# The first attention iteration reordered: embedding chain behind it, table waits ahead of it, x transposes behind the state read

## The chip, the cores and the metric

The kernel runs on one core of a Trainium2 chip. The time is device time in microseconds (us) from start to end of one execution. A core has TensorE (PE in the profile; its weight loads are PEld), VectorE (DVE), ScalarE (ACT), GpSimd (POOL) and SyncE (SP). Each works through its own list of instructions in order and meets the others at semaphores: a wait stops everything behind it on that engine. Transfers are issued by SP, ACT or POOL and run on 16 DMA engines.

## The reference

Three layers, all in float32. The data are x (8 batches, 8 heads, 512 tokens, 64) and a state of 32 rows per head.

```python
scores = scale * x @ state.T;   a = softmax(scores);   xread = a @ state
scores2 = scale * state @ x.T;  a2 = softmax(scores2); sread = a2 @ x
x = concat([xread, sread]).transpose(...).reshape(B * (S + Ns), H * D)      # 4352 rows of 512
en = expert_emb / |expert_emb|;  logits = (x / |x|) @ en.T / tau            # 8 experts
e = argmax(logits);  x = gate * (relu(x @ w1[e]) @ w2[e])
h = relu(x @ w_in);  out = (s * h * h + b) @ w_out
```

## The kernel before

The program has one stream per engine, written out by hand, and three stages: attention with routing, experts, dense layer.

**Attention.** A loop over the eight batches, `i` from 0 to 7. In iteration `i`, TensorE multiplies states by the transposed tokens (`scores`, L1263); ScalarE copies the result to `s_t`; VectorE takes its minimum `nb` (L971), ScalarE the exponential, TensorE turns it (`turn_e2`), ScalarE copies it to `a2_n` (L639), and `state_read` (L1319) multiplies it by x into `bank_r`. The other softmax goes over the turned scores in `bank_n`: VectorE subtracts the minimum, ScalarE takes the exponential (L659), VectorE sums and normalises (L994 to L1000). `x_transpose` (L1244) turns the tokens of the next batch in four pieces, two into each of two banks, and ScalarE's `x_evac` (L584) copies each to `x_t`. `token_read` of batch `i - 1` fills `x_rows`, which SP stores to `x_tok` in memory. Each iteration ends with a slice of the expert weights being split in two parts (`split_hi`, `split_lo`).

**Before the loop.** The states are turned in four groups by `st_transpose` and copied by VectorE's `evac_st` to `st_t`: group 0 ahead of the loop, the others in iteration 0. Group 3 and group 0 use `bank_r`, which `state_read` uses too. The expert embedding is normalised by a chain of 17 small steps (`embed`, the first on ScalarE at L644, the others on VectorE), turned by TensorE, and multiplied by the states (`embed_states`, L1280).

**Routing.** The logits of some batches together (groups 0,1,2 then 3,4 then 5, 6 and 7) are turned into positions: `choose` on VectorE, `ranks` on TensorE, `place` on VectorE, after which GpSimd scatters five columns of indices for each batch into `slot_tab` (L508). `ranks` of the group whose last batch is `b` runs in iteration `b + 2` and waits for the state logits of the batch before. The table is cleared first by a transfer from `zero_f` (L387), whose semaphore is `tab_cleared`. SP reads the first indices back (`idx_soon`, L400) once 25 scatters have landed, and its later stores stand behind that wait; then GpSimd gathers the rows of the first tile (L525).

**Order of transfers on SP:** x of batch 0 in eight pieces, states, x of batch 1, `w1[0]` (2 MB), x of batch 2, `w2[0]` (2 MB), two scalars, the clearing of the table, and then the loop's loads and stores.

**Waits on constants.** GpSimd makes the constants and raises `const_ready` and `tab_zero`. VectorE waits for `tab_zero` 8 (the last of GpSimd's writes) at the start of iteration 1.

Of the kernel before, what the change touches and what calls it, by code (L numbers as in the profile page):

```python
# [4 lines left out]
P = 128  # L5
# [6 lines left out]
def attention_moe_ffn(nc, x, state, emb, tau, w1, w2, w_in, w_out, s, b, out):  # L12
# [57 lines left out]
    with top:  # L70
# [400 lines left out]
        def _(pool):  # L471
# [23 lines left out]

            pool.wait_ge(tab_zero, 4)
            nc.gpsimd.memset(first_e[:], 0.0).then_inc(tab_zero, 1)
            pool.wait_ge(tab_zero, 5)
# [29 lines left out]

            pool.wait_ge(tab_cleared, 16)
            for bb in range(SOON):  # L530
# [47 lines left out]
        def _(act):  # L578
# [62 lines left out]

            x_evac(0, 0)
            act.wait_ge(emb_ready, 16)
            nc.scalar.activation(emb_sq[:], emb_sb[:], ACT.Square, accum_out=en[0:E, 0:1]).then_inc(emb_step, 1)  # L644
            for j in range(1, PAIRS):
                x_evac(0, j)
            for i in range(B):
                scores_evac(i)
                if i >= 1:
                    a1_evac(i - 1)  # L650
                exp_states(i)
                if i >= 1:
                    row_t_evac(i - 1)
                a2_evac(i)
                if i + 1 < B:
                    for j in range(2):
                        x_evac(i + 1, j)
                act.wait_ge(sh_done, i + 1)
                nc.scalar.activation(e1[:], e1[:], ACT.Exp, scale=-1.0).then_inc(e1_done, 1)  # L659
                if i + 1 < B:  # L660
                    for j in range(2, PAIRS):
                        x_evac(i + 1, j)
                if i >= 1:
                    rows_evac(i - 1)
                split_hi(i)
# [156 lines left out]
        def _(dve):  # L822
# [37 lines left out]

            def embed_turned():
                dve.wait_ge(emb_tr, 1)
                nc.vector.tensor_copy(emb_t[:], bank_l[:, L_SE:L_SE + PAIRS * E].rearrange("p (c e) -> p c e", e=E))\
                    .then_inc(emb_done, 1)

            def embed_states():
                dve.wait_ge(se_mm, 1)
                nc.vector.tensor_scalar(st_pair[:, :, :, P:P + E],
                                        bank_l[:, L_SE:L_SE + B * 2 * E].rearrange("p (b j e) -> p b j e", b=B, e=E),
                                        -1.0 / SCALE, None, ALU.mult).then_inc(se_ready, 1)  # L870
# [86 lines left out]
            e1_r = e1[:].rearrange("p t (h w) -> p (t h) w", w=NS)  # L957
            sc_r = bank_n[:].rearrange("p t (h w) -> p (t h) w", w=NS)
            dve.wait_ge(hot_zero, 5)
            embed()  # L960
            evac_st(0)
            embed_turned()
            for i in range(B):
                if i == 1:
                    dve.wait_ge(const_ready, CONSTS + 2)
                    dve.wait_ge(tab_zero, 8)
                for jj in range(2):
# [4 lines left out]
                if i >= 1:  # L972
                    a1_evac(i - 1)
                else:
                    for k in range(1, B // 2):
                        evac_st(k)
                dve.wait_ge(scN_done, i + 1)
# [24 lines left out]
                token_rows(i)  # L1002
                if i == 0:
                    embed_states()
                if i == B - 1:
# [225 lines left out]
        def _(pe):  # L1231
# [33 lines left out]

            def embed_turn():
                pe.wait_ge(emb_step, EMB_STEPS)
                for j in range(PAIRS):
                    last = nc.tensor.transpose(bank_l[:, L_SE + j * E:L_SE + (j + 1) * E], emb_n[:, j * P:(j + 1) * P], ident[0:E, 0:E])
                last.then_inc(emb_tr, 1)  # L1270

            def embed_states():
                pe.wait_ge(st_ready, B // 2)
                pe.wait_ge(emb_done, 1)
# [33 lines left out]
            def state_read(bb):  # L1308
                pe.wait_ge(a2_ready, 2 * bb + 2)
                if bb >= 1:  # L1310
                    pe.wait_ge(st_rows_ready, (P // NS) * bb)
                else:
                    pe.wait_ge(st_ready, B // 2)
                for jj in range(2):
# [74 lines left out]
            st_transpose(0)  # L1389
            embed_turn()  # L1390
            for i in range(B):
                scores(i)
                if i == 0:
                    for k in range(1, B // 2):
                        st_transpose(k)
                else:
                    turn_a1(i - 1)
                    turn_rows(i - 1)
                turn_scores(i)
                turn_e2(i)  # L1400
                if i == 0:
                    embed_states()
                else:
                    row_logits(i - 1)
                if i + 1 < B:
                    for j in range(2):
                        x_transpose(i + 1, j)
                state_read(i)
                if i + 1 < B:
                    for j in range(2, PAIRS):  # L1410
                        x_transpose(i + 1, j)
                for k in range(len(GROUPS)):
                    if GROUPS[k][-1] + 2 == i:
                        ranks(k, i)
                if i >= 1:
                    token_read(i - 1)
# [196 lines left out]
```

## Time and profile before

| | |
|---|---|
| median of 3 runs | 1444.6 us (1443.0 to 1444.9) |
| profiled execution | 1443.0 us, span from first to last instruction 1441.3 us |
| mean granted TensorE clock | 0.973 of full |
| busy | PE 1356.8 us, DVE 645.9, ACT 513.7, POOL 161.1 |
| attention and routing | to about 160 us of the span |

The share of an engine is an average over the three stages. What a change in the first stage is worth is read from that stage: the order in time of the instructions, what each waited for, and which event released the next stage.

### The profile page before, as it was taken

What the parts mean: (1) busy time and instruction counts of PE and PEld (TensorE: products, weight loads), DVE (VectorE), ACT (ScalarE), POOL (GpSimd) and SP (SyncE); (2) the same over time, 40 slices, a digit from 0 to 9 for tenths busy, and PEclk for the clock granted to TensorE, in tenths of its full rate; (3) what the DMA queues carried; (4) which work ended last, traced back from release to release, by engine and by line L of the source; (5) the groups of instructions that cost most, each with busy time, mean ns of one, the idle gap of its engine ahead of it and who ended that gap; (6) DMA issues with size and microseconds to landing.
All of it is one profiled execution on the core that took longest, in us unless ns stands there. A gap on an engine that the chain in (4) does not pass through costs nothing.

```text
span 1441.3 us, 22771 instructions
## 1 busy us (share of the span) xinstructions
PE 1356.8 (94%) x6908; PEld 1119.1 (78%) x6909; DVE 645.9 (45%) x1603; ACT 513.7 (36%) x953; POOL 161.1 (11%) x200
## 2 busy tenths in 40 slices
PE   7977579999999999997999999999999999999995
PEld 5756458888888878886888888888888888888884
DVE  5875353666664565557422423223232232322322
ACT  4864133555543454443422222222222222222221
POOL 1042410111110111115000101001010010100101
PEclk9997699999999999998999999999999999999998
DMA  9593451344441243141010100101000010000000
GB/s 252 157 110 53 84 189 38 114 165 176 142 152 45 99 166 118 45 176 44 8 37 1 59 0 19 39 0 58 0 29 29 0 58 0 32 26 0 30 0 30
DMA packets 75601, 100.20 MB, mean 70 GB/s; under 512 B 44424, under 2 KB 44968, under 8 KB 74544
## 3 DMA queue, kind: packets, MB, share of 16 engines
q1 hardware_dynamic: 62736, 69.71, 17.1%
q0 software_dynamic: 7200, 20.08, 4.2%
q10 hardware_dynamic: 5632, 9.98, 1.8%
q8 instruction: 20, 0.33, 0.1%
q14 instruction: 13, 0.11, 0.0%
HBM read 71.24 MB, written 28.66 MB: 69 GB/s over the span
## 4 chain that ended last, share of the span: by engine, by line
PE 79%; DVE 6%; DMA 4%; issue 4%; POOL 2%; ACT 1%; DVEq 1%; SPq 0%; ACTq 0%; POOLq 0%
PE bank_a L1544 26%; PE bank_n L1563 14%; PE bank_tt L1563 12%; PE bank_n L1497 11%; PE bank_a L1464 10%; DMA xg<-x_tok,g_idx 3%; POOL slot_tab L508 2%; PE bank_tt L1477 2%; DVE w_lo L1029 1%; PE bank_n L1446 1%; DMA slot_tab<-ids,pos_all 1%; DVE gc L834 1%; PE bank_a L1244 1%; DVE gc L836 1%; PE bank_r L1319 1%
## 5 line engine op out<-in xcount | busy, mean ns | idle before, releaser
L1191 DVE TENSOR_TENSOR sq<-rel 128x512 f32<-128x512 f32 (+1 forms) x144 | 95.5, 663 | 487.3 <-ACT rel L797 487.3
L797 ACT ACTIVATE rel<-bank_a 128x512 f32<-128x512 f32 (+1 forms) x144 | 82.8, 575 | 541.6 <-PE bank_a L1544 541.6
L1544 PE MATMUL bank_a<-y_hi,w_in_hi 128*128 128x512 f32 (+1 forms) x576 | 217.7, 378 | 0.1
L1544 PE MATMUL bank_a<-y_hi,w_in_lo 128*128 128x512 f32 (+1 forms) x576 | 217.3, 377 | 0.0
L1544 PE MATMUL bank_a<-y_lo,w_in_hi 128*128 128x512 f32 (+1 forms) x576 | 217.3, 377 | 0.0
L1497 PE MATMUL bank_n<-w_hi,hid_hi 128*128 128x512 f32 x296 | 118.0, 398 | 14.4 <-DVE hid_lo L1045 14.3
L1544 PEld LDWEIGHTS bank_a<-y_hi,w_in_hi 128*128 128x128 f32 x576 | 108.3, 188 | 21.4 <-issue 0.8
L1544 PEld LDWEIGHTS bank_a<-y_lo,w_in_hi 128*128 128x128 f32 x576 | 108.3, 188 | 20.7 <-issue 0.2
L1544 PEld LDWEIGHTS bank_a<-y_hi,w_in_lo 128*128 128x128 f32 x576 | 108.3, 188 | 19.9
L1497 PE MATMUL bank_n<-w_hi,hid_lo 128*128 128x512 f32 x296 | 116.9, 395 | 0.0
L568 POOL DMA_INDIRECT out_rows<-w_raw,out_id x34 | 36.5, 1074 | 691.8 <-DVE w_raw L1203 686.6
L1563 PE MATMUL bank_n<-wo_hi,g_hi 128*128 128x512 f32 x288 | 112.5, 391 | 0.7 <-DVE g_lo L1194 0.7
L1563 PE MATMUL bank_n<-wo_lo,g_hi 128*128 128x512 f32 x288 | 112.2, 390 | 0.0
L1563 PE MATMUL bank_n<-wo_hi,g_lo 128*128 128x512 f32 x288 | 112.1, 389 | 0.0
L1464 PE MATMUL bank_a<-w_hi,xg_hi 128*128 128x512 f32 x304 | 101.8, 417 | 3.4 <-DVE xg_lo L1016 2.8
L1563 PE MATMUL bank_tt<-wo_hi,g_hi 128*128 128x512 f32 x256 | 100.8, 394 | 0.0
L1563 PE MATMUL bank_tt<-wo_lo,g_hi 128*128 128x512 f32 x256 | 99.7, 389 | 0.0
L1563 PE MATMUL bank_tt<-wo_hi,g_lo 128*128 128x512 f32 x256 | 99.6, 389 | 0.0
L1194 DVE TENSOR_TENSOR g_lo<-sq,g_hi 128x512 fp32r<-128x512 f32 (+1 forms) x144 | 95.5, 663 | 6.8
L1464 PE MATMUL bank_a<-w_hi,xg_lo 128*128 128x512 f32 x304 | 97.5, 402 | 0.0
L801 ACT ACTIVATE g_hi<-rel 128x512 fp32r<-128x512 f32 (+1 forms) x144 | 87.7, 609 | 4.6
L1497 PEld LDWEIGHTS bank_n<-w_hi,hid_hi 128*128 128x128 f32 x296 | 56.7, 191 | 29.5 <-issue 15.0
(234 smaller groups left out, 2096.0 us busy)
## 6 DMA issues: line engine op xcount, KB each, us to landing
w_raw<-in_moe_w SPq DMA_DIRECT2D x16, 2048.0 KB, 9.3
moe_tok<-yg ACTq DMA_DIRECT2D x38, 256.0 KB, 2.0
x_tok<-x_rows SPq DMA_DIRECT2D x8, 1088.0 KB, 7.8
y_rows<-moe_tok SPq DMA_DIRECT2D x8, 1024.0 KB, 5.2
x_m<-in_x SPq DMA_DIRECT2D x7, 1024.0 KB, 8.4
win_raw<-in_moe_w_in SPq DMA_DIRECT2D x8, 512.0 KB, 10.6
w_raw<-in_moe_w_out SPq DMA_DIRECT2D x1, 4096.0 KB, 15.9
x_m<-in_x SPq DMA_DIRECT2D x8, 128.0 KB, 3.0
```

The costliest lines, as they stand in the source:

```text
L508: nc.gpsimd.indirect_dma_start(out=slot_tab[:, :], out_offset=bass.IndirectOffsetOnAxis(ap=pos_all[0:n, bb, t:t + 1], axis=0), in_=ids[0:n ...
L568: nc.gpsimd.indirect_dma_start(out=out[:, :], out_offset=bass.IndirectOffsetOnAxis(ap=out_id[:, r:r + 1], axis=0), in_=o_sb[:, k, :], in_o ...
L797: nc.scalar.activation(rel[:, k, 0:cols], ps_g[k][:, 0:cols], ACT.Relu).then_inc(rel_ready, 1)
L801: nc.scalar.activation(g_hi[:, k, 0:cols], rel[:, k, 0:cols], ACT.Square).then_inc(g_hi_done, 1)
L834: link(nc.vector.scalar_tensor_tensor(t, y, n2, y, ALU.mult, ALU.mult))
L1191: nc.vector.tensor_tensor(sq[:, 0:cols], rel[:, k, 0:cols], rel[:, k, 0:cols], ALU.mult).then_inc(sq_ready, 1)
L1194: nc.vector.tensor_tensor(g_lo[:, k, 0:cols], sq[:, 0:cols], g_hi[:, k, 0:cols], ALU.subtract).then_inc(g_ready, 1)
L1464: last = nc.tensor.matmul(ps_h[j][:], a[:, xc], w[:, c * F + j * BANK:c * F + (j + 1) * BANK], start=(c == 0 and a is xg_hi and w is w1_hi ...
L1477: last = nc.tensor.transpose(ps_ht[m][:, c * P:(c + 1) * P], hid[:, k * P:(k + 1) * P], ident[:])
L1497: last = nc.tensor.matmul(dst, a[:, kc], w[:, k * D:(k + 1) * D], start=(k == 0 and a is hid_hi and w is w2_hi), stop=(k == FC - 1 and w i ...
L1544: last = nc.tensor.matmul(ps_g[n % 2][:, 0:cols], w[:, wc], a[:, c, 0:cols], start=(c == 0 and w is w_in_hi and a is y_hi), stop=(c == DC ...
L1563: last = nc.tensor.matmul(ps_o[TROWS - rows + r], a[:, n % 2, rc], w[:, wc], start=(n == 0 and a is g_hi and w is wh), stop=(n == FC2 - 1 ...
```

## The change

On GpSimd the wait for `tab_cleared` moves ahead of the last four writes of constants. On VectorE the waits for `const_ready` and `tab_zero` 8 move from iteration 1 to ahead of iteration 0; `embed` and `embed_states`, now with the copy of the turned embedding in it, move to the end of iteration 0, and so does the evacuation of state group 3. On ScalarE the square of the embedding follows the first score evacuations. On TensorE the four x transposes all follow `state_read`, `ranks` precedes it, state group 3 is turned after the x transposes of iteration 0 and once the state rows have left `bank_r`, and the embedding's turn and products come after that, ahead of the scores of iteration 1. `state_read(0)` waits for one group of states instead of four.

```diff
--- before.py
+++ after.py
@@ -494,6 +494,7 @@
                            allow_small_or_imprecise_dtypes=True).then_inc(tab_zero, 1)
 
             pool.wait_ge(tab_zero, 4)
+            pool.wait_ge(tab_cleared, 16)
             nc.gpsimd.memset(first_e[:], 0.0).then_inc(tab_zero, 1)
             pool.wait_ge(tab_zero, 5)
             nc.gpsimd.memset(first_e[:, 0:1], 1.0).then_inc(tab_zero, 1)
@@ -526,7 +527,6 @@
                                              in_=x_tok[0:SOON * ROWS if isinstance(g, int) and g < EARLY else NTOK, :],
                                              in_offset=bass.IndirectOffsetOnAxis(ap=g_idx[:], axis=0)).then_inc(gathered, 16)
 
-            pool.wait_ge(tab_cleared, 16)
             for bb in range(SOON):
                 write_slots(bb)
             pool.wait_ge(soon_loaded, 16)
@@ -639,15 +639,15 @@
                     nc.scalar.activation(a2_n[:, :, jj * P:(jj + 1) * P], bank_t[jj].rearrange("p (t w) -> p t w", w=P),
                                          ACT.Copy).then_inc(a2_ready, 1)
 
-            x_evac(0, 0)
-            act.wait_ge(emb_ready, 16)
-            nc.scalar.activation(emb_sq[:], emb_sb[:], ACT.Square, accum_out=en[0:E, 0:1]).then_inc(emb_step, 1)
-            for j in range(1, PAIRS):
+            for j in range(PAIRS):
                 x_evac(0, j)
             for i in range(B):
                 scores_evac(i)
                 if i >= 1:
                     a1_evac(i - 1)
+                else:
+                    act.wait_ge(emb_ready, 16)
+                    nc.scalar.activation(emb_sq[:], emb_sb[:], ACT.Square, accum_out=en[0:E, 0:1]).then_inc(emb_step, 1)
                 exp_states(i)
                 if i >= 1:
                     row_t_evac(i - 1)
@@ -858,12 +858,10 @@
                 emb_link(nc.vector.tensor_scalar(emb_n[:], emb_sb[:], en[0:E, 5:6], inv_tau[0:E, :], ALU.mult, ALU.mult))
                 assert n_emb[0] == EMB_STEPS
 
-            def embed_turned():
+            def embed_states():
                 dve.wait_ge(emb_tr, 1)
                 nc.vector.tensor_copy(emb_t[:], bank_l[:, L_SE:L_SE + PAIRS * E].rearrange("p (c e) -> p c e", e=E))\
                     .then_inc(emb_done, 1)
-
-            def embed_states():
                 dve.wait_ge(se_mm, 1)
                 nc.vector.tensor_scalar(st_pair[:, :, :, P:P + E],
                                         bank_l[:, L_SE:L_SE + B * 2 * E].rearrange("p (b j e) -> p b j e", b=B, e=E),
@@ -956,14 +954,11 @@
 
             e1_r = e1[:].rearrange("p t (h w) -> p (t h) w", w=NS)
             sc_r = bank_n[:].rearrange("p t (h w) -> p (t h) w", w=NS)
+            evac_st(0)
+            dve.wait_ge(const_ready, CONSTS + 2)
             dve.wait_ge(hot_zero, 5)
-            embed()
-            evac_st(0)
-            embed_turned()
+            dve.wait_ge(tab_zero, 8)
             for i in range(B):
-                if i == 1:
-                    dve.wait_ge(const_ready, CONSTS + 2)
-                    dve.wait_ge(tab_zero, 8)
                 for jj in range(2):
                     dve.wait_ge(sT_ready, 2 * i + jj + 1)
                     if i >= 1:
@@ -972,8 +967,8 @@
                 if i >= 1:
                     a1_evac(i - 1)
                 else:
-                    for k in range(1, B // 2):
-                        evac_st(k)
+                    evac_st(1)
+                    evac_st(2)
                 dve.wait_ge(scN_done, i + 1)
                 nc.vector.tensor_reduce(m1[:], sc_r, X_AXIS, ALU.min).then_inc(m1_done, 1)
                 dve.wait_ge(m1_done, i + 1)
@@ -1001,6 +996,8 @@
                     .then_inc(a1_norm, 1)
                 token_rows(i)
                 if i == 0:
+                    evac_st(B // 2 - 1)
+                    embed()
                     embed_states()
                 if i == B - 1:
                     a1_evac(B - 1)
@@ -1263,14 +1260,11 @@
                         last = nc.tensor.matmul(bank_t[jj][p, :], st_t[:, i, jj, p], x_t[:, 2 * jj + par, :], start=True, stop=True)
                     last.then_inc(scT_done, 1)
 
-            def embed_turn():
+            def embed_states():
                 pe.wait_ge(emb_step, EMB_STEPS)
                 for j in range(PAIRS):
                     last = nc.tensor.transpose(bank_l[:, L_SE + j * E:L_SE + (j + 1) * E], emb_n[:, j * P:(j + 1) * P], ident[0:E, 0:E])
                 last.then_inc(emb_tr, 1)
-
-            def embed_states():
-                pe.wait_ge(st_ready, B // 2)
                 pe.wait_ge(emb_done, 1)
                 for bb in range(B):
                     for jj in range(2):
@@ -1310,7 +1304,7 @@
                 if bb >= 1:
                     pe.wait_ge(st_rows_ready, (P // NS) * bb)
                 else:
-                    pe.wait_ge(st_ready, B // 2)
+                    pe.wait_ge(st_ready, 1)
                 for jj in range(2):
                     for t in range(TPB):
                         for par in range(2):
@@ -1387,32 +1381,32 @@
                 x_transpose(0, j)
             pe.wait_ge(diag_ready, 16 * (P // NS))
             st_transpose(0)
-            embed_turn()
             for i in range(B):
                 scores(i)
                 if i == 0:
-                    for k in range(1, B // 2):
-                        st_transpose(k)
-                else:
+                    st_transpose(1)
+                    st_transpose(2)
+                if i >= 1:
                     turn_a1(i - 1)
                     turn_rows(i - 1)
                 turn_scores(i)
                 turn_e2(i)
-                if i == 0:
-                    embed_states()
-                else:
+                if i >= 1:
                     row_logits(i - 1)
-                if i + 1 < B:
-                    for j in range(2):
-                        x_transpose(i + 1, j)
-                state_read(i)
-                if i + 1 < B:
-                    for j in range(2, PAIRS):
-                        x_transpose(i + 1, j)
                 for k in range(len(GROUPS)):
                     if GROUPS[k][-1] + 2 == i:
                         ranks(k, i)
-                if i >= 1:
+                state_read(i)
+                if i + 1 < B:
+                    for j in range(PAIRS):
+                        x_transpose(i + 1, j)
+                if i == 0:
+                    pe.wait_ge(st_rows_ready, P // NS)
+                    st_transpose(3)
+                    pe.wait_ge(const_ready, CONSTS + 2)
+                    pe.wait_ge(st_ready, B // 2)
+                    embed_states()
+                else:
                     token_read(i - 1)
             turn_a1(B - 1)
             turn_rows(B - 1)
```

## Rows read from the trace of the kernel before

**Rows 1.** The page's busy time, share of the span and instructions of each engine.
```profile
PE 1356.8 (94%) x6908; PEld 1119.1 (78%) x6909; DVE 645.9 (45%) x1603; ACT 513.7 (36%) x953; POOL 161.1 (11%) x200
```

**Rows 2.** Timeline of the start: start us, us, engine, line, operation, idle before.
```profile
5.99 0.10 POOL L497 MEMSET first_e<- 128x8 f32 x1
...
6.38 0.10 POOL L502 MEMSET late<- 128x2 f32 x1
...
7.25 0.16 DVE L853 RECIPROCAL inv_tau<-inv_tau 128x1 f32<-128x1 f32 x1 [4.65 <-ACT emb_sq L644]
...
10.14 0.53 DVE L858 TENSOR_SCALAR emb_n<-emb_sb,en,inv_tau 8x512 f32<-8x512 f32 x1
...
13.54 0.18 DVE L863 COPY emb_t<-bank_l 128x32 f32<-128x32 f32 x1
...
13.77 3.68 PE L1263 MATMUL bank_tt<-x_t,st_t 128*64 128x512 f32 x8 [0.43 <-DVE st_t L841]
14.04 8.47 SPq L383 DMA_DIRECT2D w_raw<-in_moe_w  x1
...
16.41 0.69 DVE L971 TENSOR_REDUCE nb<-s_t 128x1 f32<-128x512 f32 x1 [2.69 <-ACT s_t L617]
...
21.61 2.04 PE L1280 MATMUL bank_l<-emb_t,st_t 128*64 128x8 f32 x64
...
23.94 0.91 SPq L387 DMA_DIRECT2D slot_tab<-zero_f  x1
...
32.06 1.27 DVE L971 TENSOR_REDUCE nb<-s_t 128x1 f32<-128x512 f32 x2
```

**Rows 3.** Transfers under way at 22 to 25 us, the last column us to landing.
```profile
w_raw<-in_moe_w SPq DMA_DIRECT2D x1, 2048.0 KB, 17.8
slot_tab<-zero_f SPq DMA_DIRECT2D x1, 144.0 KB, 9.7
```

**Rows 4.** Timeline of iteration 2, and rank matmuls of iteration 4.
```profile
44.73 1.27 DVE L971 TENSOR_REDUCE nb<-s_t 128x1 f32<-128x512 f32 x2
...
47.05 1.26 ACT L639 ACTIVATE a_n<-bank_tt 128x512 f32<-128x512 f32 x2
...
48.64 1.09 ACT L584 ACTIVATE x_t<-bank_a 128x512 f32<-128x512 f32 x2 [0.33 <-PE bank_a L1244]
...
48.97 1.97 PE L1319 MATMUL bank_r<-x_m,a_n 128*64 128x128 f32 x32
...
49.47 0.15 DVE L896 COPY st_rows<-bank_l 32x8 f32<-32x8 f32 x1
49.61 1.06 ACT L659 ACTIVATE e<-e 128x1024 f32<-128x1024 f32 x1
50.70 1.22 DVE L994 TENSOR_REDUCE s<-e 128x32 f32<-128x1024 f32 x1 [1.08 <-ACT e L659]
...
57.48 1.27 DVE L971 TENSOR_REDUCE nb<-s_t 128x1 f32<-128x512 f32 x2
...
78.89 0.59 PE L1380 MATMUL bank_l<-hot_g,ones_b 128*128 128x112 bf16 x14
```

**Rows 5.** Timeline of iteration 6 and its end.
```profile
100.97 1.27 DVE L971 TENSOR_REDUCE nb<-s_t 128x1 f32<-128x512 f32 x2
...
109.38 1.97 PE L1244 MATMUL bank_a<-ident,x_m 128*128 128x128 f32 x8 [5.11 <-DMA x_m<-in_x]
...
111.28 3.68 PE L1319 MATMUL bank_r<-x_m,a_n 128*64 128x128 f32 x32
...
117.61 0.98 POOL L508 DMA_INDIRECT slot_tab<-ids,pos_all  x1 [15.81 <-DVE pos_all L937]
...
119.78 0.33 SPq L392 DMA_DIRECT2D x_tok<-x_rows  x1
```

**Rows 6.** The chain that ended last, at the last scatter of group 1.
```profile
129.61 11.59 DMA slot_tab<-ids,pos_all
```

**Rows 7.** Transfers issued from 118 to 124 us, the last column us to landing.
```profile
x_tok<-x_rows SPq DMA_DIRECT2D x1, 1088.0 KB, 10.8
```

## The prediction

> **What bounds the kernel now.** I read the page's totals first [rows 1]: TensorE is busy for 94% of the span, so time is won or lost where TensorE waits, and a delay ahead of the expert and dense stages moves them whole. Then the timeline of the start [rows 2], the transfers that are on their way by then [rows 3], one plain iteration of the attention loop [rows 4], a later one that stalls [rows 5], and the hand-over from the loop to the experts: the chain [rows 6] and the store beside it [rows 7]. In the start the reader is to see that VectorE's first score reduction runs at 16.41 us and the embedding chain, 7.25 to 10.67, lies ahead of the state evacuation while TensorE waits for input. In rows 4, the reduction `nb` of one iteration at 44.73 and of the next at 57.48: a period of 12.75. In rows 6, the last slot-table scatter of group 1 lands 11.59 us after its issue and holds the chain; behind it come the early index load, the first gather and everything after it.
>
> **The change, part by part.** All times are shifts against the profiled execution (1443.0 us, span 1441.3).
>
> (a) The wait for the cleared table. GpSimd waits for the clearing transfer before its last four writes, and VectorE waits for the last of these (`tab_zero` 8) ahead of iteration 0. SyncE issues that transfer at 23.94, and no wait on computed data lies ahead of it in SyncE's queue, so the change does not move the issue [rows 2]. It takes 9.7 us to land [rows 3]: 33.6. The four writes take 6.48 - 5.99 = 0.5 [rows 2], hand-over 0.1: VectorE starts at 34.2 instead of 16.41, +17.8. Queued behind VectorE's wait are ScalarE's exponentials (they want `nb`), TensorE's transposes of `e2`, and so the state read. Low bound: the 2 MB load issued at 14.04 with 17.8 to landing [rows 2, 3] is ahead in the queue and lands at 31.8; were the clear to land with it, the term is 16.0. The Trainium skill (DMA: Bandwidth & Descriptors, Queues, rings and completion order) says that descriptors of one ring are consumed in order and that a semaphore increment lands only after earlier writes of that engine; the order of landings here agrees, and by that rule the sum cannot fall below the one with 16.0.
>
> (b) The rest of iteration 0. Before: 32.06 - 16.41 = 15.65 [rows 2]. After, from 34.2: two `nb` 1.27 (35.5), two evacuations about 0.7 each (36.9), two 1.22 passes over the scores (39.3). Meanwhile exponentials, transposes and `a_n` end 48.31 - 44.73 = 3.6 after `nb` [rows 4], plus 0.5 because TensorE has idled some 15 us and comes back at half clock: 38.3. The state read at that clock takes 3.68 [rows 5], not 1.97 [rows 4]: 42.0. The transposes of x are now behind it, all four pieces: 0.7 to the first evacuation (a quarter of the 1.97 of rows 5, and a hand-over of 0.2), 1.1 for two (43.8), exponential 1.06 (44.9). VectorE's sums, normalisation and state rows, about 4.2 of the 6.78 from 50.70 to 57.48 [rows 4]: 49.1. Only then the last state transpose and evacuation, 1.9 at low clock (51.0); the embedding chain 3.42 [rows 2] (54.4), which is covered by nothing now: ScalarE and TensorE have run out of work; turn and copy 1.0, an estimate from the 0.18 copy and four tiny transposes (55.4); 64 small matmuls, 2.04 at full clock [rows 2], 3.7 at the ratio 3.68/1.97 (59.1); scores of iteration 1, 2.64 to the first `nb` as at 13.77 to 16.41 [rows 2] (61.8), and the second bank comes 1.2 later than back-to-back `nb` would want. So 28.8 against 15.65: +13.1. If TensorE is at full clock from 54 on, 3.7 of this is not paid: +9.4. Moving the scalar square on ScalarE costs nothing, 0.8 us under VectorE's wait.
>
> (c) Iterations 1 to 5. The transposes of x no longer run while ScalarE empties `e2`, and ScalarE finds nothing ready until the state read is over. By rows 4, counted from `nb`: `a_n` 3.6, state read 5.5, first `x_t` 6.2, two of them 7.3, exponential 8.4; before, it ended at 50.67 - 44.73 = 5.9, and VectorE idled 1.08 for it. From that reduction to the next `nb` VectorE has 6.78 with about 0.8 idle in it, so the next `nb` falls 14.35 after: +1.6. Before, five iterations took 100.97 - 32.06 = 68.9 [rows 2, 5], which is five of 12.75 and 5.2 of routing. After: 71.75 + 5.2, and another 0.9 in iteration 4, where the rank matmuls (0.59 and their neighbours [rows 4]) now stand before the state read: 77.8, +8.9 (+8.0 without the last).
>
> (d) The ranks of group 1. Before, they stood behind the x transposes of iteration 6, and these waited 5.11 us for x to land and then ran at half clock (1.97 for eight) [rows 5]; GpSimd could scatter at 117.61, 16.64 after that iteration's `nb` (100.97). After, the ranks need only the state logits, ready 49.62 - 44.73 = 4.9 after `nb` [rows 4], plus 0.6 to 0.9, plus 1.0 for placing: 6.7. That is -9.9.
>
> (e) The hand-over. Sum to the last scatter's issue: 17.8 + 13.1 + 8.9 - 9.9 = +29.9. The scatters are slow to land while the 1 MB store of token rows (issued 119.78, 10.8 to landing [rows 5, 7]) uses the transfer engines. After, that store is issued about 14.1 after iteration 6's `nb`, not 18.8, so it shifts by 17.8 + 13.1 + 8.9 - 4.7 = +35.1. If only the scatters set the end, the total is +29.9; if what is queued drains behind the store, +35.1. Half of the scatters precede the store now, so I take +31.4, nearer the first.
>
> Sum: 1443.0 + 31.4 = 1474.4; the median of the three runs is 1.6 above the profiled one, so 1476. Low end of the terms: 16.0 + 9.4 + 8.0 - 9.9 = +23.5; high end: +35.1 and one more episode of low clock in the loop, some 4 (iterations 3 and 5 leave TensorE about 2 us idle each).
>
> **Rivals.**
> 1. *The hand-over gives back.* If a scatter lands soon after its issue once it no longer runs with the store, up to 9.5 of the 11.59 [rows 6] is saved there; the rows of batch 6 and their store would then end last, about 3 us under my store-free sum. Time 1444.6 + 27 = 1471, and with the low ends of (a) and (b) 1466. The Trainium skill (DMA: Bandwidth & Descriptors, Queues, rings and completion order) has each engine alternate between the rows that have work, packet by packet; the late landing in rows 6 speaks against quick passage.
> 2. *TensorE stays slow.* If it doesn't return to full clock after the idle start, each iteration's TensorE work of about 11 us grows by some 80%: seven iterations by 8 each less the idle 3, some +35, 1511. For: half clock after a 5 us wait [rows 5]. Against: in the middle of a loop that is mostly transposes the state read takes 1.97 [rows 4], its full-clock time (3.68 at half [rows 5]). The Trainium skill (TensorE: Matmul & The Clock Gate, PE-mode transpose) says that transposes don't count as work for the clock in the same way; the state read at 1.97 among them shows no harm from that.
> 3. *Faster.* The mechanism is (d): the x load of iteration 6 no longer stands before the ranks, -9.9 against +8.9 of (c), net -1.0. It decides only if the start costs nothing, which wants the cleared table at about 16 us; it lands at 33.6 [rows 3]. Time 1443.6 to 1435.
> 4. *Absorbed.* The delay vanishes before the experts because something bound to wall-clock time ends last there. I see none: each later load waits on computed data. Time 1444.6.
>
> **How the numbers follow.** Forecast 0.66, rival 1 0.17, rival 2 and partial forms of it 0.13, rival 3 0.02, rival 4 0.02. The forecast is the first case's, 1476. The range 1465 to 1486 holds the first two and the mild end of the third. 0.2% (3 us) is about what a measurement of this kernel can tell from no change. Slower by more 0.96; faster 0.02; within 0.02.
>
> **What would show it.** First `nb` at 33 to 35 us with a wait on GpSimd ahead of it; the second iteration's at 59 to 63, with state-embedding matmuls of 3 to 4 us after an idle TensorE; later `nb` steps of 14.3 or more; the scatters of group 1 starting some 7 after iteration 6's `nb`, no x wait there; the first gather 27 to 35 later than before; the stages after it of unchanged length. The prediction is wrong if the clear lands far earlier than 33, if the loop's steps stay at 12.75, or if the gather's shift is not handed on to the end.

## The result and the profile after

The changed kernel takes 1494.7 us (median of four runs, 1491.5 to 1497.5) against 1444.8 us; the ratio is 1.0342 with a 95% interval of [1.0316, 1.0370]. That is 49.9 us slower, where 31.4 were forecast and 1486 was the upper end of the range. The sign and the two largest terms were right, the sum was not.

The first reading is the timeline of the start in the changed kernel; it answers to [rows 2].

```profile
24.19 0.85 SPq L387 DMA_DIRECT2D slot_tab<-zero_f  x1
...
33.10 0.10 POOL L503 MEMSET late<- 128x2 f32 x1
33.41 1.28 DVE L966 TENSOR_REDUCE nb<-s_t 128x1 f32<-128x512 f32 x2 [19.60 <-POOL late L503]
...
37.66 3.68 PE L1313 MATMUL bank_r<-x_m,a_n 128*64 128x128 f32 x32 [0.69 <-ACT a_n L639]
...
50.38 0.16 DVE L853 RECIPROCAL inv_tau<-inv_tau 128x1 f32<-128x1 f32 x1
...
53.27 0.53 DVE L858 TENSOR_SCALAR emb_n<-emb_sb,en,inv_tau 8x512 f32<-8x512 f32 x1
...
54.86 3.59 PE L1274 MATMUL bank_l<-emb_t,st_t 128*64 128x8 f32 x64 [0.35 <-DVE emb_t L863]
...
60.92 0.69 DVE L966 TENSOR_REDUCE nb<-s_t 128x1 f32<-128x512 f32 x1 [1.01 <-ACT s_t L617]
...
62.63 0.69 DVE L966 TENSOR_REDUCE nb<-s_t 128x1 f32<-128x512 f32 x1 [1.02 <-ACT s_t L617]
```

GpSimd's last write ends at 33.2 and VectorE, idle 19.60 us, starts `nb` at 33.41 instead of 16.41. TensorE comes back at half clock (granted clock 0.50 from 35.0 to 41.3, 3.68 us for the state read against 1.97 in [rows 4]). The embedding chain, 50.38 to 53.80, stands alone, the 64 small matmuls take 3.59 at half clock (0.50), and the second `nb` of iteration 1 starts at 62.63, which in the kernel before began 0.64 after 32.06.

The loop, by VectorE's `nb` of iterations 2 to 7:

```profile
76.64 1.27 DVE L966 TENSOR_REDUCE nb<-s_t 128x1 f32<-128x512 f32 x2
...
90.61 1.27 DVE L966 TENSOR_REDUCE nb<-s_t 128x1 f32<-128x512 f32 x2
...
106.78 1.27 DVE L966 TENSOR_REDUCE nb<-s_t 128x1 f32<-128x512 f32 x2
...
125.24 1.27 DVE L966 TENSOR_REDUCE nb<-s_t 128x1 f32<-128x512 f32 x2
...
150.96 1.27 DVE L966 TENSOR_REDUCE nb<-s_t 128x1 f32<-128x512 f32 x2
...
170.95 1.27 DVE L966 TENSOR_REDUCE nb<-s_t 128x1 f32<-128x512 f32 x2
```

The steps of iterations 1 to 6 are 14.7 (from 0.64 before the 62.63 above), 14.0, 16.2, 18.5, 25.7 and 20.0 us. In the kernel before they were 12.7, 12.75, 14.3, 14.4, 14.8 and 23.6; its wait for x sat in the last of these [rows 5]. The timeline of iterations 4 and 5 of the changed kernel shows what is in the long ones:

```profile
108.37 1.36 PE L1290 MATMUL bank_tt<-ident,e 128*128 128x128 f32 x8 [2.07 <-ACT e L631]
...
111.82 0.26 PE L1372 MATMUL bank_l<-hot_g,before 128*128 128x120 bf16 x1 [1.75 <-DVE st_rows L894]
...
112.85 3.68 PE L1313 MATMUL bank_r<-x_m,a_n 128*64 128x128 f32 x32
...
114.27 1.16 POOL L509 DMA_INDIRECT slot_tab<-ids,pos_all  x1 [81.07 <-DVE pos_all L935]
...
119.56 1.22 DVE L989 TENSOR_REDUCE s<-e 128x32 f32<-128x1024 f32 x1 [5.59 <-ACT e L659]
...
134.06 0.15 DVE L893 COPY lg_all<-bank_l 32x8 f32<-32x8 f32 x1 [4.00 <-remote]
...
144.06 0.62 ACT L602 ACTIVATE x_rows<-bank_tt 128x544 f32<-128x544 f32 x1 [4.09 <-DMA x_tok<-x_rows]
144.49 1.24 DVE L886 TENSOR_TENSOR st_rows<-bank_r,r 32x128 f32<-32x128 f32 x4 [2.42 <-DMA x_tok<-st_rows]
```

Ahead of the ranks TensorE waits 1.75 us for the state logits, after 2.07 us of idle ahead of the transposes of `e`, and the state read then runs at half clock (0.50 from 112.85 to 116.5). In iteration 5 VectorE stands 4.00 us at 134.06 ("remote": the trace has no releaser for it), ScalarE waits 4.09 us and VectorE 2.42 us for stores of batch 3. There is no wait for x in iteration 6, as forecast, but there are waits for stores of about that size in iteration 5, which was not.

At the hand-over, the stall list of the changed kernel from 60 to 200 us (engine and line, waited for, us in total, times, longest) and the transfer issued from 162 to 168 us:

```profile
POOL g_idx L517 <- DMA idx_soon<-slot_tab: 25.8, 1, 25.8
ACT x_rows L602 <- DMA x_tok<-x_rows: 21.6, 3, 15.0
...
DVE st_rows L886 <- DMA x_tok<-st_rows: 11.6, 2, 9.2
```

```profile
x_tok<-x_rows SPq DMA_DIRECT2D x1, 1088.0 KB, 24.4
```

The store of batch 5 takes 24.4 us to land (10.8 in [rows 7]), `rows_evac(6)` waits 15.0 us for it, and the index load goes out at 193.8 instead of 141.2. The first gather is issued at 196.34 instead of 144.85, 51.5 us later. The third gather, which needs the rows of all eight batches, is issued at 242.56 instead of 189.54, 53.0 later; the spans differ by 53.4 and the medians by 49.9, so behind that gather hardly anything is lost.

### The profile page after: what moved, and what is told of

It reads as the page before. It is cut to its first block, busy times and chain, and to the rows that moved or that the text cites. A ratio compares the mean times of both kernels' runs of the same rounds, so it can differ in the third digit from the quotient of the medians.

```text
span 1494.7 us, 22772 instructions
## 1 busy us (share of the span) xinstructions
PE 1373.4 (92%) x6908; PEld 1129.8 (76%) x6909; DVE 646.5 (43%) x1603; ACT 512.8 (34%) x953; POOL 160.6 (11%) x200
## 4 chain that ended last, share of the span: by engine, by line
PE 77%; DMA 7%; DVE 7%; issue 3%; ACT 3%; SPq 2%; DVEq 1%; POOL 0%; ACTq 0%; POOLq 0%
PE bank_a L1538 25%; PE bank_n L1557 13%; PE bank_tt L1557 12%; PE bank_n L1491 11%; PE bank_a L1458 9%; DMA x_tok<-x_rows 3%; DMA xg<-x_tok,g_idx 3%; PE bank_tt L1471 2%; PE bank_r L1313 1%; DVE w_lo L1026 1%; PE bank_n L1440 1%; DVE gc L834 1%; DMA slot_tab<-zero_f 1%; SPq L383 1%; DVE gc L836 1%
## 5 line engine op out<-in xcount | busy, mean ns | idle before, releaser
L1491 PE MATMUL bank_n<-w_hi,hid_hi 128*128 128x512 f32 x296 | 117.9, 398 | 14.5 <-DVE hid_lo L1042 14.3
```

The costliest lines, as they stand in the source:

```text
L1491: last = nc.tensor.matmul(dst, a[:, kc], w[:, k * D:(k + 1) * D], start=(k == 0 and a is hid_hi and w is w2_hi), stop=(k == FC - 1 and w i ...
```

## The experiments

Two questions were open: what each part costs alone, and where the 18 us are that the sum lacks.

**The parts alone, on the kernel before.**

Waits only:

```diff
             pool.wait_ge(tab_zero, 4)
+            pool.wait_ge(tab_cleared, 16)
...
+            dve.wait_ge(const_ready, CONSTS + 2)
+            dve.wait_ge(tab_zero, 8)
             for i in range(B):
-                if i == 1:
-                    dve.wait_ge(const_ready, CONSTS + 2)
-                    dve.wait_ge(tab_zero, 8)
```

> Kernel before with the two waits alone moved (GpSimd waits for the cleared table ahead of its last four writes, VectorE waits for them ahead of iteration 0). My prediction's term (a): first nb near 33.5 us instead of 16.4, and 2 to 3 us more because TensorE comes back at half clock; order of scatters and stores inside the loop as before. Total +17 to +21 us. Theory Q (the 18 us that I missed come from the token-row store being issued behind the slot-table scatters, which needs the earlier ranks): the same +17 to +21, with stores landing in 10 to 20 us as before. Rival S (a late start by itself upsets the later transfers): +28 or more.

Measured 1.0167 [1.0145, 1.0190], +24 us, between the range of term (a) and that of rival S. The second iteration's `nb` is at 49.25, 17 later than before, as term (a) has it. The other 7 us appear further on:

```profile
105.32 1.36 PE L1295 MATMUL bank_tt<-ident,e 128*128 128x128 f32 x8 [0.96 <-issue]
...
110.71 1.23 DVE L977 TENSOR_REDUCE m<-bank_n 128x32 f32<-128x1024 f32 x1 [4.98 <-remote]
...
119.11 0.60 ACT L639 ACTIVATE a_n<-bank_tt 128x512 f32<-128x512 f32 x1 [12.98 <-remote]
```

ScalarE's copy of `e2` starts at 119.11 after 12.98 us of idle, though TensorE had turned both halves by 106.7. The trace shows no instruction of another engine that it still had to wait for. The queues from 116 to 118 us (packets, MB, share of 16 engines; the times of packets overlap, so a share can pass 100%) hold one instruction transfer:

```profile
q1 hardware_dynamic: 695, 0.18, 248.7%
q0 software_dynamic: 71, 0.00, 41.8%
q8 instruction: 1, 0.02, 18.2%
```

18.2% of 16 engines over 2 us is 5.8 us for that one packet of 0.02 MB; from 80 to 100 us in the changed kernel, without scatters, two such packets took 0.6% of 20 us together, 1.9 us. A sequencer that waits for its next instructions would look like this; the trace doesn't name the cause, so it stays an argument.

The embedding chain and state group 3 only (the ScalarE, VectorE and TensorE hunks that move `emb_sq`, `embed`, `embed_states`, `evac_st(3)` and `st_transpose(3)`):

```diff
                 token_rows(i)
                 if i == 0:
+                    evac_st(B // 2 - 1)
+                    embed()
                     embed_states()
```

> Kernel before with the embedding chain, its turn and products, and state group 3 alone moved behind iteration 0. My term (b) without the idle start: second iteration's nb 8 to 12 us later, handed on whole: +8 to +12 us. Theory Q: the same. Rival E (the chain is still hidden by ScalarE and VectorE work): under +4.

Measured 1.0083 [1.0060, 1.0106], +12 us: the second iteration starts at 39.92 instead of 32.06, the rest comes in the loop. Nothing hides the chain there. (The diff above shows a part of VectorE's hunk.)

The x transposes only:

```diff
-                if i + 1 < B:
-                    for j in range(2):
-                        x_transpose(i + 1, j)
                 state_read(i)
                 if i + 1 < B:
-                    for j in range(2, PAIRS):
+                    for j in range(PAIRS):
                         x_transpose(i + 1, j)
```

> Kernel before with all four x transposes behind the state read, nothing else. My term (c): steps of 14.0 to 14.4 instead of 12.75, +8 by iteration 6; the x load that iteration 6 waited 5.1 us for is less late, so +4 to +9 at the end. Theory Q: the same range, as the ranks stay where they were. Rival (free, because another engine sets the step): 0 to +2.

Measured 1.0094 [1.0074, 1.0114], +13 us. Its plain steps are 14.0 us. The upper end of the expectation is passed; the profile has one step of 27.9 us (iteration 5), where the longest in the kernel before is 23.6.

The ranks only:

```diff
+                for k in range(len(GROUPS)):
+                    if GROUPS[k][-1] + 2 == i:
+                        ranks(k, i)
                 if i + 1 < B:
                     for j in range(2):
                         x_transpose(i + 1, j)
```

> Kernel before with ranks alone moved ahead of the x transposes and the state read. My prediction's term (d): scatters of group 1 start 7 to 10 us earlier and the end moves with them, -1 to -10 us. Theory Q: those earlier scatters are in flight when the token rows are stored; the store takes 20 us or more instead of 10.8, the row buffer is released late, and the gain is lost: 0 to +12 us.

Measured 1.0091 [1.0061, 1.0121], +13 us where my term (d) had up to -10. This is the step of the prediction that failed with the wrong sign. VectorE's `nb` of iterations 4 to 7 in it:

```profile
70.68 1.27 DVE L971 TENSOR_REDUCE nb<-s_t 128x1 f32<-128x512 f32 x2
...
92.99 0.67 DVE L971 TENSOR_REDUCE nb<-s_t 128x1 f32<-128x512 f32 x1
97.20 0.69 DVE L971 TENSOR_REDUCE nb<-s_t 128x1 f32<-128x512 f32 x1 [3.54 <-issue]
...
115.82 1.27 DVE L971 TENSOR_REDUCE nb<-s_t 128x1 f32<-128x512 f32 x2
...
142.61 1.27 DVE L971 TENSOR_REDUCE nb<-s_t 128x1 f32<-128x512 f32 x2
```

Iteration 3 has not changed; iteration 4, where the first scatters go out, has grown from 14.4 to 26.5 (70.68 to 97.20, the second of the pair), and iteration 6 still takes 26.8.

**Parts taken out of the changed kernel.** Ranks back behind the x transposes:

```diff
-                for k in range(len(GROUPS)):
-                    if GROUPS[k][-1] + 2 == i:
-                        ranks(k, i)
                 state_read(i)
                 if i + 1 < B:
                     for j in range(PAIRS):
                         x_transpose(i + 1, j)
+                for k in range(len(GROUPS)):
+                    if GROUPS[k][-1] + 2 == i:
+                        ranks(k, i)
```

> Changed kernel with ranks alone put back behind the x transposes. Theory Q: the scatters start after most of the iteration's work, few are in flight when the store is issued, the store lands in about 10 us again: 8 to 14 us faster than the changed kernel, about 1481 to 1487. My prediction's term (d) taken at its word: 8 to 10 us slower than the changed kernel, about 1504.

Measured 1.0289 [1.0253, 1.0325] against 1.0342, 7.7 us faster than the changed kernel. The direction is theory Q's, the size just under its range of 8 to 14, and the two intervals overlap. The step of iteration 4 is 16.65 instead of 18.46, that of iteration 5 is 33.1 instead of 25.7. GpSimd's wait for the table back behind the constants:

```diff
             pool.wait_ge(tab_zero, 4)
-            pool.wait_ge(tab_cleared, 16)
...
+            pool.wait_ge(tab_cleared, 16)
             for bb in range(SOON):
```

> Changed kernel with GpSimd's wait for the cleared table alone put back behind the constants. My term (a): first nb near 16.5 us again, TensorE not idle, so 17 to 22 us faster than the changed kernel: 1473 to 1478. Rival A (the start is then held by another wait moved ahead of iteration 0, the constants or group 3): less than 10 us faster.

Measured 1.0213 [1.0186, 1.0239], 18.7 us faster than the changed kernel, first `nb` at 16.54. Term (a) holds in both directions.

**Is it the order of store and scatters?** Theory Q said that the stores land late because they are issued behind scatters. So GpSimd was made to wait for the store:

```diff
             def write_slots(bb):
                 pool.wait_ge(pos_ready, ...)
+                if bb in (GROUPS[0][0], GROUPS[1][0]):
+                    pool.wait_ge(rows_stored, 16 * (GROUPS[0][-1] + 2 if bb == 0 else GROUPS[1][-1] + 2))
```

> Changed kernel, but GpSimd waits for the token-row store of the iteration (batch 3 for group 0, batch 5 for group 1) before it scatters a group. Theory Q: both stores land in 5 to 7 us instead of 21 and 24, iteration 5 falls from 25.7 to about 16 to 17 us; the scatters of group 1 start some 13 us later, so the net is 5 to 15 us faster than the changed kernel. Rival S (the long landings are not the scatters' doing): iteration 5 keeps 25 us and the later scatters add 10: 1505.

> Kernel before with the same wait for the store ahead of the scatters of groups 0 and 1. Theory Q: the stores that took 9.8 and 19.6 us land in 5 to 10, the 5 us wait for x in iteration 6 shrinks only if the load is ahead of the scatters too; group 1 starts some 8 us later: -6 to +6 us. Rival S: +8.

Measured: changed kernel 1.0381 [1.0353, 1.0410], about 6 us slower still, though the intervals overlap; kernel before 1.0082 [1.0054, 1.0110], +12 us. Theory Q's ranges were missed in both. Rival S's 1505 was met in the changed kernel (1504.6), but what rival S says, that the long landings are not the scatters' doing, does not stand up to the runs with the scatters held back, further on. With the store out of the way iteration 5 takes 29.7 us in the one and 31.1 in the other, and ten scatters need 25.0 us (175.3 to 200.3) and 24.8 us (133.24 to 158.08) from the first issue to the index load, as in the kernel before (117.61 to 141.22, 23.6), though no store was issued among them. The scatters are slow to land by themselves, and which transfer came first matters less. Theory Q is dropped in that form.

**Without the contention.** All 25 early scatters held back until the last state read:

```diff
+            pool.wait_ge(sread_done, B)
             for bb in range(SOON):
                 write_slots(bb)
```

> Kernel before, but GpSimd holds the 25 scatters of groups 0 and 1 back until the last state read. All work is done, only later, so the whole time says nothing; what counts are the nb steps and whether any engine stands still without a recorded releaser. Theory Q2 (while scatters are in flight everything that shares the transfer engines lands late: stores, x loads, instruction refills): steps of 12.7, 12.7, 14.3, 14.4, about 14.5 and 15 to 16, no wait for x in iteration 6, x load of batch 7 in 8 us instead of 25.5. Rival S (the long step comes from somewhere else): one step above 20 remains.

> The same in the changed kernel. Theory Q2: steps of 14.0, 14.0, 16.2, 16.5, 16.0 and 17.7, as my term (c) has them, stores in 5 us, no step above 19; the last nb is then 27 to 31 (start and embedding) plus 9 to 13 later than in the kernel before with the same hold. Rival P (half-clock episodes in TensorE are what I missed): steps of 18 and more remain without any scatter.

Measured, one run each: 1474.2 and 1522.7 us, 48.4 apart. The last `nb` is 45.8 us later, above the 36 to 44 that was expected. The `nb` of iterations 4 to 7 in the kernel before and then of iterations 2 to 7 in the changed one, both with the hold:

```profile
71.35 1.27 DVE L972 TENSOR_REDUCE nb<-s_t 128x1 f32<-128x512 f32 x2
...
85.77 1.28 DVE L972 TENSOR_REDUCE nb<-s_t 128x1 f32<-128x512 f32 x2
...
99.79 1.27 DVE L972 TENSOR_REDUCE nb<-s_t 128x1 f32<-128x512 f32 x2
...
115.51 1.27 DVE L972 TENSOR_REDUCE nb<-s_t 128x1 f32<-128x512 f32 x2
```

```profile
77.16 1.28 DVE L967 TENSOR_REDUCE nb<-s_t 128x1 f32<-128x512 f32 x2
...
91.14 1.27 DVE L967 TENSOR_REDUCE nb<-s_t 128x1 f32<-128x512 f32 x2
...
107.30 1.27 DVE L967 TENSOR_REDUCE nb<-s_t 128x1 f32<-128x512 f32 x2
...
125.73 1.27 DVE L967 TENSOR_REDUCE nb<-s_t 128x1 f32<-128x512 f32 x2
...
141.60 1.27 DVE L967 TENSOR_REDUCE nb<-s_t 128x1 f32<-128x512 f32 x2
...
161.30 1.27 DVE L967 TENSOR_REDUCE nb<-s_t 128x1 f32<-128x512 f32 x2
```

The steps are 14.4, 14.0 and 15.7 in the one, and 14.0, 16.2, 18.4, 15.9 and 19.7 in the other. No step above 20 is left; the x load of batch 7 lands in 9.2 and 9.1 us instead of 25.5 and 27.9. Iteration 7 starts 45.8 us later in the changed kernel (161.30 - 115.51) with no scatter in flight. The difference of the two kernels is nearly the same with the contention out of the loop (48.4, from one run each, so good to a few us) as with it (49.9). The hold takes away two things at once, though: the contention, and whatever the earlier ranks gain, since the scatters leave after the last state read in both kernels. Equal differences therefore say that what the change adds in contention and what its earlier ranks gain cancel within a few us, not that both are nothing: without the hold iteration 6 begins 50.0 us late, with it 41.8 (141.60 - 99.79). The 3.68 us state reads of iterations 4, 6 and 7 are there in the held version as well (granted clock 0.50), so rival P holds for a part.

What the contention costs can now be read from iterations 4 to 7. With the hold they take 115.51 - 71.35 = 44.2 and 161.30 - 107.30 = 54.0 us. To see how much of the rest belongs to one execution, both kernels were profiled again.

> The kernel before again, for a second profile. If its loop is as the first profile has it: iteration 6 at 23 to 25 us with the wait for x, and 23 to 25 us from the first scatter of group 1 to the index load. If single executions differ: one of the two numbers moves by more than 3 us.

> The changed kernel again, unchanged, for a second profile. If the 36 us from the first scatter of group 1 (157.8) to the index load (193.8) belong to the kernel, the second profile has 33 to 38 us there and a step of 24 to 28 in iteration 5; if they are a matter of the single execution, 24 to 28 us there.

```profile
70.80 1.27 DVE L971 TENSOR_REDUCE nb<-s_t 128x1 f32<-128x512 f32 x2
...
85.22 1.28 DVE L971 TENSOR_REDUCE nb<-s_t 128x1 f32<-128x512 f32 x2
...
110.33 1.27 DVE L971 TENSOR_REDUCE nb<-s_t 128x1 f32<-128x512 f32 x2
...
119.12 0.97 POOL L508 DMA_INDIRECT slot_tab<-ids,pos_all  x1 [18.68 <-DVE pos_all L937]
...
126.05 1.27 DVE L971 TENSOR_REDUCE nb<-s_t 128x1 f32<-128x512 f32 x2
```

```profile
106.37 1.27 DVE L966 TENSOR_REDUCE nb<-s_t 128x1 f32<-128x512 f32 x2
...
136.03 1.28 DVE L966 TENSOR_REDUCE nb<-s_t 128x1 f32<-128x512 f32 x2 [0.67 <-issue]
...
153.21 1.27 DVE L966 TENSOR_REDUCE nb<-s_t 128x1 f32<-128x512 f32 x2
...
178.69 1.34 DVE L966 TENSOR_REDUCE nb<-s_t 128x1 f32<-128x512 f32 x2
```

The same program puts the long step in another iteration: before, iteration 6 (23.6) in one profile and iteration 5 (25.1) in the other; changed, iteration 5 (25.7), then iterations 4 (29.7) and 6 (25.5). The toll above the held versions is 8.6 and 11.1 us before (52.8 and 55.25 less 44.2), 10.2 and 18.3 changed (64.2 and 72.3 less 54.0). The time from the first scatter of group 1 to the index load also moves: 23.6 and 24.9 before, 36.0 and 27.7 changed. The whole times of the two changed profiles are 1496.6 and 1496.3 all the same. The first gather does not decide that by itself: it is at 196.34 in one and at 190.90 in the other, but the third gather is at 242.56 and 242.14; iteration 7 began 7.7 us later in the second (178.69 against 170.95). The 36 us were of that execution.

The second profile of the kernel before also shows what the early ranks are worth without a wait for x in iteration 6: its first scatter of group 1 goes out 8.8 us after that iteration's `nb` (119.12 - 110.33), against 6.9 in the second profile of the changed kernel (160.08 - 153.21). That is 1.9 us, where the first pair of profiles has 9.8. The profile that I read before predicting is the one with the smallest toll seen here, 8.6.

**Attempts at a better version.** Each x load one place earlier in SyncE's list:

```diff
-                if bb + 3 < B:
-                    load_x(bb + 3)
+                if bb == 0:
+                    load_x(3)
+                if bb + 4 < B:
+                    load_x(bb + 4)
```

> Kernel before with each x load issued one place earlier in SyncE's list (ahead of the wait for the token rows of the iteration before), so the load of batch 7 goes out near 78 us, ahead of the first scatter at 81.5. Theory Q2: it lands in about 8 us, the 5.1 us wait in iteration 6 and the half-clock work behind it vanish: 3 to 10 us faster than before. Rival (the contention only moves to the stores and instruction refills): 0 to 10 us slower.

> The same in the changed kernel: the load of batch 7 goes out near 117 us, after the first scatters at 114.3 in either case, ahead of the store by some 6 us. Theory Q2: the load still shares the engines with the scatters, so -5 to +5 us against the changed kernel. Rival (the load is the whole of the missing time): 10 to 18 us faster.

Measured 0.9994 [0.9983, 1.0006] and 1.0328 [1.0311, 1.0345]: no difference before, and 2 us under the 1.0342 of the changed kernel. The 2 us are well inside the intervals. In the kernel before the wait for x is gone, and iteration 5 takes 25.3 us instead. The second profile of the unchanged kernel looks the same (25.1 in iteration 5), so the edit need not have moved the toll; removing one wait for it gained nothing, and that is the prediction's error in small. Smaller groups on the kernel before, `GROUPS = ((0, 1), (2, 3), (4,), (5,), (6,), (7,))`:

> Kernel before with the routing groups (0,1), (2,3), (4) in place of (0,1,2), (3,4). Batch 4's five scatters are then all that is left for iteration 6; ten scatters took 24 us from the first issue to landing, five should take 12: the index load and the first gather 8 to 12 us earlier, less 1 us for one more ranking, total 5 to 11 us faster than before. Rival (the ten scatters of batches 2 and 3, in iteration 5 and 6, hold x, stores and refills as long as the 15 did later): within 3 us of before.

Measured 1.0024 [1.0010, 1.0037], slower by 3 us, as the rival had it. The ten scatters of batches 2 and 3 went out at 99.5 to 111.5, those of batch 4 at 124.9 to 130.1, and the index load at 147.2: the stalls came earlier, and the last five needed 22.3 us from the first issue to the index load, where 12 were expected and ten had taken 23.6. No version beat the kernel before.

## Why the prediction was wrong, point by point

- **(a) the cleared table, +17.8:** measured +17.0 (33.41 for 16.41). The clear took 8.4 us to land, not 9.7. Taking the wait back out gave 18.7 us.
- **(b) embedding behind iteration 0, +13.1:** from the first `nb` to the second one of iteration 1 went 29.2 us (33.41 to 62.63), against 16.3 (16.41 to 32.70): +12.9. The low-clock steps were as forecast, 3.59 for the matmuls where 3.7 were put.
- **(c) the loop, +8.9:** with nothing in flight, iterations 1 to 5 took 79.0 us in the changed kernel (62.6 to 141.60) and 68.15 before (31.64 to 99.79, from the same pair of profiles): +10.9. (The second kernel's first `nb` of iteration 1 is put 0.64 before its second, at 62.6.) Of this, iterations 1, 2, 3 and 5 gained 1.9, 1.2, 1.9 and 1.9 where I had 1.6 each, and iteration 4, with the ranks in it, 4.0 (18.4 against 14.4) where I had 2.5. The term was mis-sized there. The 0.9 that I put for the ranks held their matmuls, but neither the 1.75 us wait for the state logits ahead of them nor the half clock of that iteration's state read (3.68 us). With the ranks moved back the step is 16.65 and the state read still takes 3.31, so the ranks cost 1.8 of it, and the half clock does not come from them alone.
- **(d) the ranks of group 1, -9.9: the step that failed.** Measured inside iteration 6 it is right to 0.1: the first scatter went out 6.86 us after `nb` (157.82 - 150.96), before 16.64. But I took the wait for x and the half clock behind it as a cost of one place, which the new order avoids, and counted it as saved. It is a toll that comes with the scatters, and it falls in another place from one execution to the next. Between the second profiles, where the kernel before has no wait for x in iteration 6, the same move is worth 1.9 us. Iteration 6 began 50.0 us late, not 39.8, since the changed kernel paid most of the toll in iteration 5, ahead of the point where I took the credit; the scatters started +40.2 instead of +29.9. The ranks moved alone cost 13 us instead of gaining.
- **(e) the hand-over, +1.5:** +12.4 in the first profile (the index load shifts by 193.8 - 141.2 = 52.6, the first scatter by 40.2), +2.8 between the second profiles (27.7 against 24.9). As a mechanism it was wrong: ten scatters take 25 us to land with no store among them. My rival 1, that they land at once without the store, is refuted by the same rows.
- **Sum without (d):** 17.0 + 12.9 + 10.9, and 4.0 for iteration 6 (19.7 against 15.7), is 44.8; with the hold 45.8 was measured at iteration 7, and there the four terms are 17.6, 13.4, 10.9 and 4.0. Iteration 6's own 4.0 stands nowhere in my sum. By this pair, in which the credit of (d) cannot arise, 9.9 of the 18.5 us that the forecast lacks are that credit, 4.0 are iteration 6 and 2.0 the rest of the loop. The whole difference is 48.4 with the hold and 49.9 without. Of the last 2.6 in the held pair 0.6 arises before the first scatter (124.16 and 170.59), 0.8 between it and the first gather (172.24 and 219.42), and 1.2 behind that.
- **Rival 2**, TensorE slow throughout, did not happen (1.97 for the state read of iterations 1 to 3, granted clock 1.00), but its partial form did, in iterations 4, 6 and 7. The loop is not mostly transposes, as I wrote: in the iteration of [rows 4] they are 6.0 of 13.1 us of matmul records. Transposes among the work did not prevent full clock (granted clock 1.00 from 45.5 to 48.9 in the kernel before, a stretch of transposes but for one group of eight small matmuls), so what the Trainium skill says of them (TensorE: Matmul & The Clock Gate, PE-mode transpose) did not show here. **Rivals 3 and 4** did not happen.

The parts alone add up to 24 + 12 + 13 + 13 = 62 us, the whole is 50. Iterations 4 to 7 took 60.6 us in the version with the waits alone and 71.9 with the ranks alone, against 52.8 and 55.3 in the two profiles of the kernel before, so some of the single changes bring a larger toll of their own. That this is why the parts don't add up is an argument; no run holds the scatters back in the single changes.

## What to carry to other kernels

Before a wait seen in a profile is entered as a saving, ask what makes the transfer late. If it is traffic that the change doesn't remove, the lateness may be paid at another place, as it was here, and little of the credit is left (1.9 of 9.9 us between the second profiles). Holding the traffic back until the stage is over, in both kernels, costs two runs and shows what an order costs without contention (it also hides what an earlier start of that traffic gains); a second profile of the unchanged program tells which of its stalls may be reasoned from at all.

A wait at the head of an engine's list costs its whole lateness even if what it guards is needed more than 100 us later; the two constants of GpSimd's last four writes, `first_e` and `late`, for which VectorE waited until 33 us, are first used at 175.5 and 181.4 us in the kernel before.

## What the runs showed of the hardware

Scatters of single words are slow beyond their issue: GpSimd issued one in 1.28 us, and ten took 23.6 to 28.6 us from first issue to landing, 36.0 in one profile; five took 22.3 with smaller groups; 25 held back took 45.5 us (124.16 to 169.65). While they are in flight a 1 MB load takes 25.5 to 32.7 us instead of 6 to 9 (15.3 in one that was issued behind the last scatter of its group), a store of 1.06 MB up to 24.4 instead of 5.

The engines are hardly busy with the scatters themselves. In the kernel before with the hold, the 25 scatters are 800 packets and took 1.3% of the 16 engines' time from 125 to 169 us; from 157 to 169.6 no packet moved at all, and the index load that waits for their landing went out at 169.65. In the changed kernel no packet moved from 173 to 177, with a token-row store issued at 166.97 still on its way. Where loads and stores are on the engines together with scatters, it is their own packets that take longer: from 84 to 109 in the kernel before the scatters took 2.8% of the engines' time, and the 2.77 MB of the other transfers 111.5%, some 160 us of engine time for a MB (25 x 16 x 1.115 / 2.77); from 83 to 93 with the hold 2.23 MB took 84.0%, some 60 for a MB. What delays them, and what the landing waits for while no packet moves, no run here shows.

The Trainium skill (DMA: Bandwidth & Descriptors, Queues, rings and completion order) has an engine serve its rows in turn, packet by packet; that a handful of word-sized writes goes with megabyte transfers this late is more than that rule would lead one to expect, and these runs show only that it happens.

Stalls without a releaser stand on ScalarE or VectorE between 60 and 200 us in most of these profiles: 14.5 us in the changed kernel with the ranks moved back, 13.6 with the x transposes alone, 13.0 with the waits alone, 7.2 in the second profile of the kernel before, none in its first and none in the changed kernel with the scatters held back (each the longest of that profile's loop). From 10 to 60 us, before any scatter, the profiles of the kernel before and of the changed one have none. Instruction transfers held in the same way would explain them, and that was not tested.
